# Another order of VectorE's work in the first phase of a fused attention and mixer kernel, with GpSimd making w1's low parts

## The reference, cut to what matters

```python
# attention: batch 4, heads 8, seq 768, head_dim 48
for t in range(S):
    state = alpha[:, :, t, :, None] * state + np.einsum('bhd,bhe->bhde', k[:, :, t], v[:, :, t])
    y[:, :, t] = np.einsum('bhd,bhde->bhe', q[:, :, t], state)
x = y.transpose(0, 2, 1, 3).reshape(B, S, H * D)
# first mixer: U 768x32, V 32x768, w_ch1 384x1536, w_ch2 1536x384
h = x.transpose(0, 2, 1) @ U @ V
u = x + h.transpose(0, 2, 1)
x = u + np.maximum(u @ w_ch1, 0.0) @ w_ch2
# second mixer: w_in 384x1024, w_spatial 768x768, w_out 512x384
h = np.maximum(x @ w_in, 0.0); u, v = h[..., :512], h[..., 512:]
v_n = (v - mean(v)) / sqrt(var(v) + 1e-6)
out = (u * (w_spatial @ v_n + b_spatial)) @ w_out
```

## Time and profile before

| | |
|---|---|
| median of 3 runs | 751.29 us (748.86 to 752.21) |
| the profiled execution | 749.4 us, of which its span is 747.6 us |
| PE busy | 711.8 us (95% of the span) |
| DVE busy | 346.3 us (46%) |
| ACT busy | 327.8 us (44%) |
| POOL busy | 202.6 us (27%) |
| PE's busy tenths in the first five of 40 slices | 1, 6, 8, 8, 8; 9 in nearly all after |

### The profile page before, as it was taken

The page is one execution under the profiler, slowest core; times in us unless marked ns, Lnnn a source line. Parts: engine busy times, 40 slices in busy tenths (PEclk is TensorE's granted clock), DMA queues, the critical chain, the costliest instruction groups (busy, mean ns, idle before and its releaser), DMA issues.

```text
span 747.6 us, 25682 instructions
## 1 busy us (share of the span) xinstructions
PE 711.8 (95%) x11408; PEld 673.2 (90%) x11408; DVE 346.3 (46%) x612; ACT 327.8 (44%) x570; POOL 202.6 (27%) x142
## 2 busy tenths in 40 slices
PE   1688899999999999999999999999999999999998
PEld 1578798999898999999999899999999998999998
DVE  5888664645654644764552412116315323431531
ACT  4887446454636445536434322225134232432412
POOL 5404480310450310350220422231330250132031
PEclk9779999999999999999999999999999999999999
DMA  9514501320401220401000332140021002001001
GB/s 290 185 41 139 166 5 38 110 65 8 141 7 35 78 87 17 141 3 41 34 4 3 96 127 63 54 147 12 1 71 57 1 33 95 0 0 63 0 0 63
DMA packets 15693, 47.12 MB, mean 63 GB/s; under 512 B 1681, under 2 KB 8081, under 8 KB 15089
## 3 DMA queue, kind: packets, MB, share of 16 engines
q1 hardware_dynamic: 15600, 45.73, 19.0%
HBM read 36.29 MB, written 9.44 MB: 61 GB/s over the span
## 4 chain that ended last, share of the span: by engine, by line
PE 89%; DVE 4%; issue 1%; ACT 1%; DVEq 0%
PE HB L832 26%; PE ZB L832 9%; PE ZB L909 7%; PE ZB L911 7%; PE ZB L910 7%; PE SB L832 6%; PE SB L709 4%; PE ZB L945 3%; PE HB L945 3%; PE SB L814 2%; PE SB L945 2%; PE SB L823 2%; PE HB L950 2%; PE ZB L950 2%; PE SB L769 1%
## 5 line engine op out<-in xcount | busy, mean ns | idle before, releaser
L1432 DVE SCALAR_TENSOR_TENSOR hid_lo<-HB,hid_hi 128x384 fp32r<-128x384 f32 x96 | 53.4, 557 | 145.0 <-ACT hid_hi L1137 144.2
L1137 ACT ACTIVATE hid_hi<-HB 128x384 fp32r<-128x384 f32 x96 | 47.2, 492 | 157.7 <-PE HB L832 157.5
L832 PE MATMUL HB<-uh,w1h 128*128 128x384 f32 x288 | 103.2, 358 | 2.6 <-DVE ul L1428 1.5
L909 PE MATMUL ZB<-hid_hi,w2h 128*128 128x384 f32 x288 | 98.6, 342 | 0.0
L832 PE MATMUL HB<-ul,w1h 128*128 128x384 f32 x288 | 96.9, 336 | 0.0
L911 PE MATMUL ZB<-hid_lo,w2h 128*128 128x384 f32 x288 | 96.7, 336 | 0.0
L832 PE MATMUL HB<-uh,w1l 128*128 128x384 f32 x288 | 96.6, 335 | 0.0
L910 PE MATMUL ZB<-hid_hi,w2l 128*128 128x384 f32 x288 | 96.3, 334 | 0.0
L662 POOL TENSOR_TENSOR gl<-gated,gh 128x384 fp32r<-128x384 f32 x32 | 32.5, 1015 | 179.6 <-ACT gh L1152 179.6
L992 ACT COPY Qd<-Q 48x768 f32<-48x768 f32 x84 | 73.0, 869 | 14.7 <-PE SB L709 5.7
L622 POOL TENSOR_TENSOR Q<-Q,bk 112x768 f32<-112x768 f32 x13 | 24.8, 1909 | 175.8 <-ACT Qd L992 175.8
(11 more groups left out here) (232 smaller groups left out, 1468.6 us busy)
## 6 DMA issues: line engine op xcount, KB each, us to landing
Q<-in_q SPq DMA_DIRECT2D x8, 672.0 KB, 6.5
AL<-in_al SPq DMA_DIRECT2D x7, 672.0 KB, 4.5
K<-in_k SPq DMA_DIRECT2D x7, 672.0 KB, 4.7
Vt<-in_v SPq DMA_DIRECT2D x8, 576.0 KB, 4.0
mid<-x2s SPq DMA_DIRECT2D x8, 576.0 KB, 4.2
x<-mid SPq DMA_DIRECT2D x4, 1152.0 KB, 5.8
out<-o_sb SPq DMA_DIRECT2D x24, 192.0 KB, 1.8
x2s<-in_w SPq DMA_DIRECT2D x9, 384.0 KB, 5.5
```

Source lines behind the costliest of these rows:

```text
L832: last = nc.tensor.matmul(dst, weights(x, w), moving(y, m), start=(n == 0 and x == y == 0), stop=(n == total - 1 and y == 1))
L909: nc.tensor.matmul(bank, w2h[:, i, cols], hi, start=(i == 0), stop=False)
L1137: nc.scalar.activation(hid_hi[:, i % HID, :], HB[i % 2][:, 0:TILE], ACT.Relu).then_inc(h_hi, 1)
L1432: nc.vector.scalar_tensor_tensor(hid_lo[:, i % HID, :], HB[i % 2][:, 0:TILE], 0.0, hid_hi[:, i % HID, :].bitcast(F32), ALU.max, ALU.subtra ...
```

## The change

Seven edits, all of them in what runs before or shortly after the first phase. (1) DVE's `first_queries(0, 2)` and `(1, 2)` stand behind the level before and no longer inside of the other group's level. (2) The totals 4 to 6 of piece (0, 1) stand behind (1, 2) and no longer behind (0, 1). (3) `square_copies` of group 0 go behind its own level 7, those of group 1 behind `key_copies`. (4) The three parts of `split_v` go behind the whole first phase, and right behind them `att_start(1, 0)`, the seven totals of the next piece, which stood behind unit u5. (5) w1's six low parts go from DVE to POOL, where they wait for the last scaling of piece (0, 1)'s queries. (6) ACT's second spread of piece (1, 0) is cut in two halves, behind h0 and behind h1. (7) SP loads the queries of (1, 0) ahead of w2's first three pieces.

```diff
@@ -201,8 +201,6 @@
-LOW1 = {(1, KV_STEP): [0, 1, 2, 3], (1, AV_STEP + 1): [4], (1, AV_STEP + 2): [5]}
-SPLIT_V = {(1, LEVELS - 1): [0], (0, T_STEP): [1], (1, KV_STEP): [2]}
@@ -561,10 +559,10 @@
             sp.wait_ge(ld_k[0], 32)
+            load_queries(1, 0, False)
+            sp.wait_ge(ld_q[0], 32)
             for n in range(W1_PIECES, W1_PIECES + STAGE):
                 load_piece(n)
-            load_queries(1, 0, False)
-            sp.wait_ge(ld_q[0], 32)
             load_values(1, 0)
@@ -634,7 +632,7 @@
             def split_low(n):
-                pool.wait_ge(w_hi, n + 1 - STAGE)
+                pool.wait_ge(w_hi, n + 1 if n < W1_PIECES else n + 1 - STAGE)
@@ -674,7 +672,9 @@
-            pool.wait_ge(w_lo, W1_PIECES)
+            pool.wait_ge(q_ready[GROUPS - 1], LEVELS - 1)
+            for n in range(W1_PIECES):
+                split_low(n)
             for n in range(W1_PIECES, W1_PIECES + STAGE):
                 split(n)
@@ -1199,7 +1199,8 @@
                         att_start(1, 0, False)
-                        att_second(1, 0)
+                    if b == 0 and kind == "h" and i < 2:
+                        att_second(1, 0, [i])
@@ -1364,9 +1359,6 @@
                     dve.wait_ge(tot_ready[g], R + n - 1)
-                    if first and n == 2 and g == 0:
-
-                        first_queries(1, n)
                     scale_k(a, g, n)
@@ -1498,28 +1490,27 @@
             for n in range(1, MASKED):
                 for g in range(GROUPS):
-                    if (g, n) == (0, 2):
-                        first_queries(0, n)
                     for piece in range(vector_pieces(n)):
                         att_piece(0, g, n, piece, True)
-                    if (g, n) == (0, 1):
+                    if g == 0 and n in (1, 2):
+                        first_queries(n - 1, 2)
+                    if (g, n) == (1, 2):
                         totals(0, 1, range(4, LEVELS - 1))
             for g, n in LAST_STEPS:
...
-                if (g, n) == (1, MASKED):
-                    for h in range(GROUPS):
-                        square_copies(h, QUARTERS[2:])
+                if (g, n) == (0, LEVELS - 1):
+                    square_copies(0, QUARTERS[2:])
                 if (g, n) == (0, T_STEP):
                     key_copies(g)
+                    square_copies(1, QUARTERS[2:])
                 if n == KV_STEP:
                     first_queries(g, LEVELS - 1)
-                for m in LOW1.get((g, n), []):
-                    split_low(m)
-                for part in SPLIT_V.get((g, n), []):
-                    split_v(part)
+            for part in range(3):
+                split_v(part)
+            att_start(1, 0)
...
                     low(b, kind, i)
-                    if b == 0 and (kind, i) == ("u", NU - 1):
-                        att_start(1, 0)
```

More of the change, by code:

```diff
@@ L987, in _, with spread @@
         def _(act):
-            def spread(a, g, n, first):
-                for hh in range(2):
+            def spread(a, g, n, first, parts=range(2)):
+                for hh in parts:
                     r = slice(hh * ROW1, hh * ROW1 + HD)
@@ L1006, in att_start, with att_second @@
                 spread(a, g, 0, first)
-            def att_second(a, g):
+            def att_second(a, g, parts=range(2)):
                 pa, pg = before(a, g)
@@ L1013, in att_second @@
                     act.wait_ge(zeroed_q[0], 2)
-                spread(a, g, 1, False)
+                spread(a, g, 1, False, parts)
             def first_spread(g, n):
@@ L1334, in key_copies @@
                                           ).then_inc(aux_act[g], 1)
-            def split_low(n):
-                dve.wait_ge(w_hi, n + 1)
-                _, hi, lo = WEIGHTS1[n]
-                nc.vector.tensor_tensor(lo, slot(n)[0], hi.bitcast(F32), ALU.subtract).then_inc(w_lo, 1)
             def att_piece(a, g, n, piece, first):
```

## The result

The changed kernel takes **769.95 us** (median of 4 runs, 765.19 to 771.01) against 751.23 us (median of 4, 748.86 to 752.21): a ratio of 1.0245 [1.0218, 1.0271], slower. The profiled execution took 770.35 us with a span of 768.6, 21.0 more than the span of before.

The account below looks back on a forecast made before the run. PE was taken to bound the kernel, with 89% of the last chain. 14.3 at xu_sb, 0.5 up to the second scores and 1.5 for the clock made 16.3 on 749.4: 765.7, say 765.5; range 752.5 to 771.

Parts of the forecast that it names:

- Step A: Levels 1 to 3: K's scaling and three totals wait for POOL, level 3's mask copy later, +4.0 (+1.0 to +5.5).
- Step B: End of the first phase: key copies and PE's KV products come earlier, -1.1 us (-1.0 to -1.4).
- Step C: Ahead of xu_sb: V's operations and totals wait for POOL; 18.5 us behind the last query scaling, xu_sb +14.3 in all.
- a rival of 5.5 us: In the queue ahead of xu_sb: one-input casts do not wait for POOL, 5.5 us less; no separate chance given.
- Step D: Up to batch 1's second scores: half of the second spread stands behind the second hidden unit, +0.5 us (0 to +1).
- Step E: Behind PE's gap of some 10 us ahead of xu_sb: some 3 us of work at the low clock, +1.5 (0 to +3).
- the forecast, 761 to 771: Whole kernel: the main case, slower, at 761 to 771 us, chance 0.60.
- DVE did not ride through: Rival ahead of xu_sb: DVE keeps SBUF across its operations, no cost there, 752.8 us; 0.16 together with no effect.
- the queue was no shorter: Rival ahead of xu_sb: casts pass or POOL waits for w2's piece, 5.5 or 3 less or both, 755 to 761; 0.20.

Follow-up runs that it names:

- the kernel with the levels alone: The kernel before with only edits (1) and (2), the moved first_queries and totals 4 to 6: 756.09 us, ratio 1.0071.
- the third experiment: The kernel before with only edit (3), the key copies, and V's three parts together behind the first phase on DVE: 753.56 us, ratio 1.0025.
- the fills: The changed kernel with w1's low parts left out, six zero fills on GpSimd that write without reading instead: 761.02 us, ratio 1.0119.
- POOL held off: The changed kernel with GpSimd starting w1's low parts only behind the seven totals of the next piece: 762.42 us, ratio 1.0152.

## Why the prediction was right

**Step A, +4.0: measured +4.4** (6.6 less the 2.2 of the start; the same 4.4 in the kernel with the levels alone, and 4.9 in the time of the one with them undone). The mechanism is the one worked out: the K scaling ends just behind POOL (28.14, 2.28 us) and the totals lose two turns. PE waited 3.9 for K behind it. In the time of the kernel with the levels alone the price reads 5.3 by the ratio, and its interval takes in 4.4.

**Step B, -1.1: measured -1.15** (5.40 less 6.55). The two profiles compare well only since the clock had risen by then in both: with the same order, but a later rise, this stretch took 22.4 to 23.1 us in four others, instead of 21.0 here and 22.2 before. In the kernel before, alone, the step gave nothing in the time, as the third experiment shows.

**Step C, 18.5 behind the last query scaling: measured 16.95.** The queue was the one foreseen: nine waits, for seven of POOL's subtractions and two of its casts (7 x 1.84 + 2 x 0.82 = 14.5). Only the free ones were others: V_hi's first cast and the first total as foreseen, but the last total instead of V's last cast. The term that was mis-sized is DVE's own work beside the waits: 4.95 less 0.1 for each wait was put on top, and 2.4 were measured (16.95 less 14.5), so each wait hides about 0.3 of DVE's operation and not 0.1. That casts of one input wait was the assumption with a rival of 5.5 us beside it; 1.78 for 0.35 and 2.06 for 0.55 settle it, and the fills show the reason. xu_sb: +14.3 predicted, 15.2 less 2.2 measured, 13.0.

**Step D, +0.5: measured +0.6** (first to second scores 7.88 against 7.31). But its price was read against the totals at their old place. Against the new one it is 1.4, which the totals' move would else have won.

**Step E, +1.5: measured +1.2** (xu_sb to first scores 7.37 against 6.16). The size is right, the way to it was luckier: not 3 us but 6.2 pass at the low clock (82.53 to 88.7), the stretch from the first `mixed` to the first scores is 1.9 longer (6.69 against 4.83), and 0.65 comes back since PE no longer waits for ACT's last rounding of xu_sb behind DVE's (0.68 instead of 1.33 from one to the other).

**What was missing** are two terms of 4.0 together. First, the clock falls a second time in the gap ahead of the second scores: +2.3. The prediction asked of the clock only behind the 10 us gap and took PE as free of trouble from 80 us on; the gap there, 1.57 before, had become 3.52. Second, a scaling of K took 4.10 us (three operations of POOL passed it), where the like one at 97.45 before took 2.24, and PE stood still ahead of level 6's scores, where it ran through before:

```profile
116.72 4.10 DVE L1250 TENSOR_TENSOR K<-K,small 112x768 f32<-112x768 f32 x1
...
120.92 1.04 PE L757 MATMUL SB<-Q,K 48*32 48x32 f32 x96 [1.51 <-issue]
```

Behind the third scores the changed kernel is 1.7 longer than before, and 1.5 of that is this wait. It is no accident of one execution: eight of the other twelve profiles have it too, 4.09 to 4.15 for the scaling and 1.50 to 1.55 for PE, while the kernel before and four variants (the levels, the key copies and the spread split alone, POOL held off) have 2.20 to 2.31 and no wait. What decides between the two is not shown.

The sum of 16.3 came out as 18.8: the missing 4.0, less 1.5, which is step C's miss with the small ones of A, D and E about cancelling. That the time lies in the forecast, 761 to 771, is in part luck: the two missing terms brought it to 769.95, 1 us under the upper edge, and step C's surplus kept it there. The rivals fell: DVE did not ride through, and the queue was no shorter.

## What to carry to other kernels

Before moving work to an idle GpSimd, list what VectorE does in those microseconds: short operations on SBUF lose a whole GpSimd instruction each, so a chain of tiny dependent steps beside as many long ones costs the long ones: here nine waits made 14.5 us. Work with one input in PSUM is what to put beside it: before, the scalings of K with decays in PSUM kept their 0.95 at 34.73 and 36.39, beside POOL's scalings of 33.62 and 35.68. A shift that ends in a gap of TensorE can cost more than the gap, so look at the granted clock behind every gap that grows, the small ones too. And where one execution is all that a trace shows, lay it against the times of the others before its waits are taken for the price.

## What the runs showed of the hardware

- A waiting VectorE operation is not next in line: most let one GpSimd instruction pass, some three (4.10 us at 116.72), and one cast three or four short fills (2.92 us). All of these had POOL's next instruction ready to go.
- Up to its first change in the records the granted clock reads 1.00 even where it can't be that: in the changed kernel 96 score matmuls take 1.51 us at 38.81 under a reading of 1.00, and 1.03 us at 89.22. Early in the span the length of a known group tells the clock better.
- The clock's rise at the end of the first phase comes at different moments in executions with nearly the same order. The ten transposing matmuls of K took 1.18 us in the profiles of before and after and in four others, 2.13 in seven and 1.88 in one. In the kernels with the changed kernel's order up to there, the stretch from the mask copy of level 3 to the KV products is 1.3 to 2.0 us longer than in the changed kernel where they took 2.13. This may be part of why single runs of one kernel lie 3 to 4 us apart; no run here tests that.
